# Attention and two MLP layers on one core: the order of the weight loads, where the first pair's rotated rows lie, which engine splits the first weights, and the order of transposes and scores in chunk 0

## The reference

```python
q_rot, k_rot = rotate(q), rotate(k)          # x1*cos - x2*sin, x1*sin + x2*cos over halves of 64
scores = matmul(q_rot, k_rot^T) / 8          # per batch and head, 576 x 576
attn = exp(scores - max(scores))
attn = attn / (sum(attn) + 1e-9)
x = (attn @ v), heads side by side           # 1152 tokens x 512
h = x @ w_in;  x = (h * sigmoid(h)) @ w_out               # 512 -> 2048 -> 512
h = x @ w2_in; x = where(h > 0, h, exp(min(h,0)) - 1) @ w2_out
```

## Time and profile before

| | |
|---|---|
| median of 3 runs | 583.98 us |
| the profiled execution's own time | 582.42 us |
| its span in the trace | 580.6 us |
| TensorE (PE) busy | 541.5 us, 93% |
| VectorE (DVE) busy | 295.8 us, 51% |
| ScalarE (ACT) busy | 349.8 us, 60% |
| GpSimd (POOL) busy | 346.2 us, 60% |
| DMA | 77.16 MB, mean 133 GB/s |

### The profile page before, as it was taken

The page is one execution under the profiler, slowest core; times in us unless marked ns, Lnnn a source line. Parts: engine busy times, 40 slices in busy tenths (PEclk is TensorE's granted clock), DMA queues, the critical chain, the costliest instruction groups (busy, mean ns, idle before and its releaser), DMA issues.

```text
span 580.6 us, 9268 instructions
## 1 busy us (share of the span) xinstructions
PE 541.5 (93%) x3308; PEld 529.8 (91%) x3308; DVE 295.8 (51%) x505; ACT 349.8 (60%) x726; POOL 346.2 (60%) x284
## 2 busy tenths in 40 slices
PE   1586789999999999999999999999999999999998
PEld 1576779999999999999999999999999999999997
DVE  4669965663336775325664425776434550047500
...
GB/s 239 185 190 174 158 197 73 174 112 193 156 114 137 137 90 164 146 102 144 129 109 140 112 108 111 109 76 114 143 103 98 145 128 128 128 109 128 124 157 28
DMA packets 43229, 77.16 MB, mean 133 GB/s; under 512 B 5296, under 2 KB 12848, under 8 KB 43184
## 3 DMA queue, kind: packets, MB, share of 16 engines
...
...
## 4 chain that ended last, share of the span: by engine, by line
PE 74%; DVE 14%; ACT 5%; issue 3%; DMA 2%; POOL 1%; SPq 0%; ACTq 0%; DVEq 0%; POOLq 0%
PE banks L895 60%; PE banks L860 4%; PE banks L832 4%; PE banks L818 3%; PE banks L820 2%; DVE neg_max L612 2%; DVE banks L686 2%; DVE act_buf L684 2%; ACT act_buf L487 1%; DVE pt_lo L619 1%; ACT prob L435 1%; DMA k_st<-k_raw 1%; PE banks L839 1%; DMA k_raw<-k 1%; DVE g_lo L619 1%
## 5 line engine op out<-in xcount | busy, mean ns | idle before, releaser
L321 POOL TENSOR_TENSOR w_lo<-w_raw,w_hi 128x512 fp32r<-128x512 f32 x192 | 247.0, 1288 | 204.3 <-ACT w_hi L475 203.6
L475 ACT CAST w_hi<-w_raw 128x512 fp32r<-128x512 f32 x189 | 117.1, 621 | 40.3 <-PE banks L895 36.2
L895 PE MATMUL banks<-x_lo,w_hi 128*128 128x384 f32 x384 | 130.5, 340 | 1.0 <-DVE g_lo L692 0.7
L895 PE MATMUL banks<-g_lo,w_hi 128*128 128x384 f32 x384 | 129.0, 336 | 0.0
L895 PE MATMUL banks<-x_hi,w_lo 128*128 128x384 f32 x384 | 128.6, 335 | 0.0
L895 PE MATMUL banks<-g_hi,w_lo 128*128 128x384 f32 x384 | 128.5, 335 | 0.0
L895 PE MATMUL banks<-x_hi,w_hi 128*128 128x384 f32 x384 | 128.5, 335 | 0.0
L895 PE MATMUL banks<-g_hi,w_hi 128*128 128x384 f32 x384 | 128.4, 334 | 0.0
L619 DVE TENSOR_TENSOR pt_lo<-banks,pt_hi 128x512 fp32r<-128x512 f32 x60 | 41.3, 689 | 94.7 <-ACT pt_hi L443 94.3
L818 PE MATMUL banks<-k_st,q_one 128*128 128x288 f32 x160 | 53.3, 348 | 30.9 <-DVE q_two L666 14.2
L435 ACT ACTIVATE prob<-banks,neg_max 128x576 f32<-128x576 f32 x72 | 53.5, 743 | 45.9 <-DVE neg_max L612 45.6
...
## 6 DMA issues: line engine op xcount, KB each, us to landing
...
k_raw<-k SPq DMA_DIRECT2D x7, 576.0 KB, 4.2
k_st<-k_raw SPq DMA_DIRECT2D x28, 144.0 KB, 2.5
...
```

The source lines that it names most:

```text
L321: nc.gpsimd.tensor_tensor(w_st[LO][:, slot, :], w_raw[:, slot, :], w_st[HI][:, slot, :].bitcast(F32), ALU.subtract).then_inc(w_lo_done, 1)
L475: nc.scalar.copy(w_st[HI][:, slot, :], w_raw[:, slot, :]).then_inc(w_hi_done, 1)
L895: last = nc.tensor.matmul(dst, w_st[wp][:, slot, m * P:(m + 1) * P], src[xp][:, tile, :], start=start and n == 0, stop=stop and n == 2)
```

## The change

1. SP: the four weight units are requested right after `load_values(0)`, ahead of q and k of pair 2. Those now wait only until the first pair is rotated (`first_q_roped`, `first_k_roped`). `place(p+1, 1)` stands ahead of `load_values(p+1)`.
2. First pair: VectorE writes the rotated rows to PSUM (keys in banks 2 and 3, queries in bank 5) and the halves are made from there. Head 1's halves are made ahead of tile 0, not after it. The second copy of the queries' hi half reads the first one. New waits: transposes of tile 1 (bank 5) wait for `first_q_lo` 2, the first end transpose (bank 2) for `first_k_lo` 2.
3. POOL starts on pair 1 once the first queries are multiplied (`first_q_scaled` 2). It makes the hi halves of the first three weight units, which VectorE did. `rope_queries(5)` stands after the three `weight_lo`.
4. ScalarE: `queries_hi(p+1)`, `keys_hi(p+1)`, `values_hi(p)` at t = 0, 1, 2 of the even heads. For pairs 2 to 4 that is three tiles later for the queries and two for the keys. `widen_sums` and `output_hi` stand in the odd heads.
5. VectorE: `row_sum` has a second column that holds 1e-9, and `sum_eps` is a reduction over the two (TENSOR_REDUCE) in place of an addition (TENSOR_SCALAR).
6. TensorE in chunk 0: the transposes of tile n stand ahead of the scores of tile n+2. After chunk 0, five of the first MLP k-tiles (3 matmuls each) stand ahead of `value_products(7)`, not three, and two rather than three stand between it and `spread_sums`; `add_outputs(6)` stands ahead of `invert_sums(3)` on VectorE.

```diff
@@ -63,7 +63,8 @@
         neg_max = sb("neg_max", [P, 2])
-        row_sum = sb("row_sum", [P, 2, QN, 2])
+        row_sum = sb("row_sum", [P, 2, QN, 2, 2])
         sum_eps = sb("sum_eps", [P, QN, 2])
@@ -96,6 +97,10 @@
+        first_keys = banks[:, 2:4, 0:HALF]
+        first_queries = banks[:, 5, 0:CT]
@@ -145,7 +150,7 @@
         ident_zero, ident_ready = sem("ident_zero"), sem("ident_ready")
-        q_zero, pads_zero = sem("q_zero"), sem("pads_zero")
+        q_zero, eps_set, pads_zero = sem("q_zero"), sem("eps_set"), sem("pads_zero")
         k_scaled, q_scaled = sem("k_scaled"), sem("q_scaled")
@@ -182,21 +187,22 @@
         def _(sp):
-            def raw_free(r, first_lo):
+            def raw_free(r, first_roped):
                 if r == 2:
-                    sp.wait_ge(first_lo, 2)
+                    sp.wait_ge(first_roped, 1)
                 elif r > 2:
...
             def load_keys(r):
-                raw_free(r, first_k_lo)
+                raw_free(r, first_k_roped)
                 sp.dma_start(k_raw[r % 2][:, :, :], k[r * P:(r + 1) * P, :].rearrange("p (a n) -> p a n", a=2)) \
...
             def load_queries(r):
-                raw_free(r, first_q_lo)
+                raw_free(r, first_q_roped)
                 sp.dma_start(q_raw[r % 2][:, :, :], q[r * P:(r + 1) * P, :].rearrange("p (a n) -> p a n", a=2)) \
@@ -239,14 +245,14 @@
             load_values(0)
+            for n in range(RING):
+                load_unit(n)
             load_queries(2)
             load_keys(2)
-            for n in range(RING):
-                load_unit(n)
             for p in range(4):
                 place(p + 1, 0)
+                place(p + 1, 1)
                 load_values(p + 1)
-                place(p + 1, 1)
                 load_queries(p + 3)
@@ -312,6 +318,10 @@
+            def first_weight_hi(n):
+                pool.wait_ge(w_in[n], 16)
+                nc.gpsimd.tensor_copy(w_st[HI][:, n, :], w_raw[:, n, :]).then_inc(first_w_hi, 1)
@@ -333,7 +343,7 @@
-            pool.wait_ge(first_q_lo, 1)
+            pool.wait_ge(first_q_scaled, 2)
@@ -349,16 +359,19 @@
             keys_lo(1)
-            for p in range(3):
+            values_lo(0)
+            for p in range(1, 4):
+                rope_queries(p + 1)
+                rope_keys(p + 1)
+                queries_lo(p + 1)
+                if p > 1:
+                    first_weight_hi(p - 2)
+                keys_lo(p + 1)
                 values_lo(p)
-                rope_queries(p + 2)
-                rope_keys(p + 2)
-                queries_lo(p + 2)
-                keys_lo(p + 2)
-            values_lo(3)
-            rope_queries(5)
+            first_weight_hi(2)
             for n in range(AHEAD):
                 weight_lo(n)
+            rope_queries(5)
             rope_keys(5)
@@ -403,13 +416,14 @@
                 act.wait_ge(first_k_roped, 1)
-                nc.scalar.mul(k_st[rows, par, :], k_raw[0][rows, 0, :], SCALE).then_inc(first_k_hi, 1)
+                nc.scalar.mul(halves(k_st[rows, par, :]), first_keys[rows, :, :], SCALE).then_inc(first_k_hi, 1)
...
                 act.wait_ge(first_q_roped, 1)
-                nc.scalar.copy(q_one[par][rows, 0:CT], q_raw[0][rows, 0, :]).then_inc(first_q_hi, 1)
-                nc.scalar.copy(q_one[par][others, 0:CT], q_raw[0][rows, 0, :]).then_inc(first_q_hi, 1)
+                nc.scalar.copy(q_one[par][rows, 0:CT], first_queries[rows, :]).then_inc(first_q_hi, 1)
+                act.wait_ge(first_q_hi, 2 * par + 1)
+                nc.scalar.copy(q_one[par][others, 0:CT], q_one[par][rows, 0:CT].bitcast(F32)).then_inc(first_q_hi, 1)
@@ -433,7 +447,7 @@
                 nc.scalar.activation(halves(prob[:, n % 3, :]), scores(n), ACT.Exp, bias=neg_max[:, n % 2:n % 2 + 1],
-                                     accum_out=row_sum[:, i // 2 % 2, t, i % 2:i % 2 + 1]).then_inc(exp_done, 1)
+                                     accum_out=row_sum[:, i // 2 % 2, t, i % 2, 0:1]).then_inc(exp_done, 1)
@@ -521,8 +535,10 @@
-            first_keys_hi(0)
-            first_queries_hi(0)
+            for par in range(2):
+                first_keys_hi(par)
+            for par in range(2):
+                first_queries_hi(par)
             for n in range(H * QN):
@@ -533,26 +549,18 @@
                     copy_out_lo(i - 2)
-                if i == 0:
+                if i % 2 == 0:
                     if t == 0:
-                        first_keys_hi(1)
-                        first_queries_hi(1)
+                        queries_hi(p + 1)
                     if t == 1:
-                        queries_hi(1)
+                        keys_hi(p + 1)
                     if t == 2:
-                        keys_hi(1)
-                if i % 2 == 0:
-                    if t == 1:
                         values_hi(p)
-                    if t == 2 and p:
+                elif p:
+                    if t == 0:
                         widen_sums(p - 1)
-                else:
-                    if t == 0 and p < 3:
-                        queries_hi(p + 2)
-                    if t == 2 and p:
+                    if t == 2:
                         output_hi(p - 1)
-                    if t == 2 and p < 3:
-                        keys_hi(p + 2)
             probs_hi(H * QN - 1)
@@ -628,7 +636,9 @@
                 dve.wait_ge(exp_done, 2 * QN * (p + 1))
-                nc.vector.tensor_scalar(sum_eps[:, :, :], row_sum[:, p % 2, :, :], EPS, None, ALU.add) \
+                if p == 0:
+                    dve.wait_ge(eps_set, 1)
+                nc.vector.tensor_reduce(sum_eps[:, :, :], row_sum[:, p % 2, :, :, :], AXES.X, ALU.add) \
                     .then_inc(eps_done, 1)
@@ -656,19 +666,15 @@
                 dve.wait_ge(first_k_hi, par + 1)
-                nc.vector.scalar_tensor_tensor(k_st[others, par, :], k_raw[0][rows, 0, :], SCALE,
-                                               k_st[rows, par, :].bitcast(F32), ALU.mult, ALU.subtract) \
+                nc.vector.scalar_tensor_tensor(halves(k_st[others, par, :]), first_keys[rows, :, :], SCALE,
+                                               halves(k_st[rows, par, :].bitcast(F32)), ALU.mult, ALU.subtract) \
                     .then_inc(first_k_lo, 1)
                 rows = rows_of[par]
-                dve.wait_ge(first_q_hi, 2 * par + 2)
-                nc.vector.tensor_tensor(q_two[par][rows, 0:CT], q_raw[0][rows, 0, :],
+                dve.wait_ge(first_q_hi, 2 * par + 1)
+                nc.vector.tensor_tensor(q_two[par][rows, 0:CT], first_queries[rows, :],
                                         q_one[par][rows, 0:CT].bitcast(F32), ALU.subtract).then_inc(first_q_lo, 1)
-            def first_weight_hi(n):
-                dve.wait_ge(w_in[n], 16)
-                nc.vector.tensor_copy(w_st[HI][:, n, :], w_raw[:, n, :]).then_inc(first_w_hi, 1)
@@ -712,29 +718,28 @@
                 nc.vector.memset(q_two[par][other_rows_of[par], :].bitcast(F32), 0.0).then_inc(q_zero, 1)
+            nc.vector.memset(row_sum[:, :, :, :, 1:2], EPS).then_inc(eps_set, 1)
             dve.wait_ge(sin_in, 16)
             dve.wait_ge(k_in[0], 16)
-            nc.vector.tensor_tensor(k_raw[0][:, 1, :], k_raw[0][:, 1, :], table[:, 1, :], ALU.mult) \
+            nc.vector.tensor_tensor(first_keys, halves(k_raw[0][:, 1, :]), halves(table[:, 1, :]), ALU.mult) \
                 .then_inc(first_k_scaled, 1)
             dve.wait_ge(first_k_scaled, 2)
-            nc.vector.tensor_tensor(k_raw[0][:, 0, :], k_raw[0][:, 0, :], k_raw[0][:, 1, :], ALU.add) \
+            nc.vector.tensor_tensor(first_keys, first_keys, halves(k_raw[0][:, 0, :]), ALU.add) \
                 .then_inc(first_k_roped, 1)
             dve.wait_ge(q_in[0], 16)
-            nc.vector.tensor_tensor(q_raw[0][:, 1, :], q_raw[0][:, 1, :], table[:, 1, 0:CT], ALU.mult) \
+            nc.vector.tensor_tensor(first_queries, q_raw[0][:, 1, :], table[:, 1, 0:CT], ALU.mult) \
                 .then_inc(first_q_scaled, 1)
             dve.wait_ge(first_q_scaled, 2)
-            nc.vector.tensor_tensor(q_raw[0][:, 0, :], q_raw[0][:, 0, :], q_raw[0][:, 1, :], ALU.add) \
+            nc.vector.tensor_tensor(first_queries, first_queries, q_raw[0][:, 0, :], ALU.add) \
                 .then_inc(first_q_roped, 1)
-            first_keys_lo(0)
-            first_queries_lo(0)
+            for par in range(2):
+                first_keys_lo(par)
+                first_queries_lo(par)
             max_tile(0)
...
                 max_tile(n + 1)
-                if n == 0:
-                    first_keys_lo(1)
-                    first_queries_lo(1)
                 if n:
@@ -749,12 +754,10 @@
                         output_lo(p - 1)
-                if n in (11, 13, 15):
-                    first_weight_hi((n - 11) // 2)
             probs_lo(H * QN - 1)
             end_lo(H - 1)
+            add_outputs(H - 2)
             invert_sums(H // 2 - 1)
-            add_outputs(H - 2)
```

(19 more changed lines are left out.)

## The result

The changed kernel takes 568.18 us (median of 4 runs, 567.37 to 568.68), the kernel before 584.29 in the same comparison: a ratio of 0.9732, 95% interval 0.9703 to 0.976. The two profiled executions took 582.42 and 568.11 us, 14.3 apart.

What follows compares the result with a forecast made beforehand. Bound: PE later; in the first 87 us, PE's waits for a queued key DMA and late VectorE maxima. From 582.42, gains 7.9+4.8+0.5=13.2 give 569.2; plus 1.56 (profiled run under median), 570.8 us; range 565.5 to 578.0.

Steps and rivals of the forecast that it cites:

- Part A: Start to tile 6's scores: these come at 23.3 us instead of 31.22, 7.9 us gained, bounds 6.1 and 9.5.
- Part B: Tile 6's to tile 24's scores: pace from 2.41 to about 2.15 us per tile, 4.8 us gained, bounds 0 and 6.9.
- The cap: Tiles 6 to 24: POOL's work and its chain with ScalarE limit the pace to 2.03 to 2.06 us per tile.
- What is taken off VectorE: Tiles 6 to 24: 3.72 us of weight copies and 1.4 us of sum_eps excess leave VectorE, 5.1 us.
- The ten waits for exp come from VectorE: PE's ten waits for exp, 10.6 us in all, arise because VectorE makes the row maxima late.
- about 1 us of that goes: After PE's gap before tile 6, 3 us ran at 1.2 rather than 2.4 GHz; about 1 us saved.
- Transposes ahead: Chunk 0: transposes before scores spare ScalarE a 0.62 us wait after each value_products, seven times, up to 3.5 us.
- R1: Tiles 6 to 24: POOL's tie to ScalarE's later order keeps pace 2.4, no gain there; 575.6 us, chance 0.20.
- Part C: Into the MLP: addition wait covered and the chain before the last k-tile shortened, 0.5 us gained, bounds 0 and 1.
- R3: Key placings for tiles 12, 18, 24 queue behind loads, each stopping PE 2.8 us; 579.2 us, chance 0.07.
- R4: Early weights are served beside pair 1's keys, making them 1.8 us late; 572.6 us, chance 0.08.
- R2: More is cashed: 2.03 us per tile from tile 6 to 24, 1 us into the MLP; 568.2 us, chance 0.15.

Runs made afterwards that it cites:

- b1: Kernel before with only the four weight units requested ahead of q and k of pair 2: 582.41 us, ratio 0.9972.
- b3: Kernel before with the weights requested ahead and ScalarE's order of hi halves as in the changed kernel: 576.03 us, ratio 0.988.
- p1: Changed kernel with POOL rotating only 288 of 576 key columns for pairs 2 to 4: 568.28 us.
- b2: Kernel before with the first three weight units' hi halves on POOL and sum_eps by reduction: 582.78 us, ratio 0.9982.
- u4: Changed kernel with the hi halves of the first three weight units back on VectorE: 570.08 us.
- u5: Changed kernel with the row sums' 1e-9 added by TENSOR_SCALAR again: 569.32 us.
- u3: Changed kernel with the scores of tile n+2 ahead of the transposes of tile n again: 572.14 us.
- u8: Changed kernel with the tail of chunk 0 (MLP k-tiles, last sums, head 6's addition) ordered as before: 569.16 us.

## Why the prediction was right, and where it was not

The forecast was 570.8 us in the median and 569.2 for a profiled execution; 568.18 and 568.11 were measured. The added 1.56 us did not apply: the changed kernel's profiled execution lies at its median, while that of before was in the lower half of runs that spread from 580.80 to 586.50. That is over half of the miss.

**Part A** (7.9 forecast, 8.63 measured). The chain came as worked out, each step up to 0.6 us early and tile 6's scores 0.7: tile 0's scores 11.35 (11.7 forecast), POOL on pair 1 at 9.25 (9.8), its keys' lo half done at 18.85 (19.4), the key pieces issued at 19.36 (19.9), exp(4) at 20.93 (21.4). PE was already at its higher level for tile 4's transposes, which I had at the lower. The cause was half told: I put's 6.1 us on the queue alone. b1 shows that this edit alone gives 1.3 us (1.1 of it at tile 6), for ScalarE's wait stood right behind it. The sum held because it walked both sides of the new kernel up to tile 6, and so included edit 4 without giving it its price; that price is 3.5 us up to tile 6 (b3 against b1).

**Part B** (4.8 forecast, 5.03 measured; 2.135 us per tile against 2.15). The size was right, and by luck: a sum of parts that came to 10 was cut down by a cap that does not exist.

- The cap is the step that failed: "something else is late next: POOL", at 2.03 to 2.06 us per tile. p1 takes 5.9 us off POOL and nothing moves.
- "What is taken off VectorE", 5.1 us "in a stretch where VectorE was full", was priced at all of its busy time. In the 16 tiles from 8 to 24 it gives 1.31 us alone (b2), and its two halves, undone one at a time in the changed kernel, cost 1.55 (u4) and 1.34 (u5). "The ten waits for exp come from VectorE" was half of the reading: the chain of the kernel before runs through POOL and ScalarE from 38.7 to 44.0 us, and through VectorE mostly from 47 on.
- The clock was read rightly and priced low: "about 1 us of that goes", and 1.55 went.
- "Transposes ahead" was bounded at 3.5 us. Undone, it costs 2.3 in this stretch and 1.85 in the 16 tiles (u3).
- Edit 4 was counted as a burden (R1). It is a release, though mostly before this stretch and in its first two tiles; in the 16 tiles its order is worth 0.9 us (b3 against b1).
- The POOL copy took 0.61 us, where I took 1.2 with bounds of 0.8 and 1.6; the GPSIMD Engine Reference of the Trainium skill (Engine selection: one-input operations run roughly at line rate) had led to 0.6, and this trace agrees with it.

**Part C** (0.5 forecast, 1.00 measured, 1.0 in u8). Both waits were read rightly; the second was under-counted.

**The rivals.** R1's placings at tiles 12, 18 and 24 never made PE wait; at tile 18 the key pieces went out at 43.69 and 44.20 for scores at 47.96. R3 fell with it. R4 fell: pair 1's keys were rotated from 12.25 on, without a wait for their DMA. R2's sum, 568.2, is the time that was measured, but not for its reason: its pace of 2.03 us per tile was not reached (2.135). The 2.6 us between it and the forecast are 0.7 more in part A, 0.2 in part B and 0.5 in part C, less the 0.36 given back later, and the 1.56 that did not apply.

**What stays open.** The undone parts add up to 25.6 us (2.4+3.6+11.6+4.0+1.9+1.1+1.0) for a gain of 16.1, so the edits have no prices of their own. POOL's early start on pair 1 was never undone alone, nor was the early making of head 1's halves; b3, which has neither, nor edits 2 and 6, still needs 2.8 us more from tile 0 to tile 6 than the changed kernel. What holds 2.135 us per tile now was not isolated. The chain there changes between ScalarE, PE and the maximum from tile to tile; POOL is excluded by p1, one engine alone by nothing.
